# Rows of q and k doubled on the host, the first bit rows ahead of other loads, products with V in two threes, and the first low weight parts on VectorE

## The reference

```python
q_bits = (np.einsum('bhsd,dk->bhsk', q, proj) > 0)
k_bits = (np.einsum('bhsd,dk->bhsk', k, proj) > 0)
mask = q_bucket[:, :, :, None] == k_bucket[:, :, None, :]
scores = scale * np.matmul(q, k.transpose(0, 1, 3, 2))
scores = np.where(mask, scores, -1000000000.0)
attn = np.exp(scores - np.max(scores, axis=-1, keepdims=True))
attn = attn / (np.sum(attn, axis=-1, keepdims=True) + 1e-09)
attn_out = np.matmul(attn, v)
...
for e in range(E):        # first mixture: the expert of the largest cosine to x
    mask = expert_idx == e
    out[mask] = gate_w[mask, None] * (np.maximum(x[mask] @ w1[e], 0.0) @ w2[e])
...                       # second mixture: the same over the two best noisy logits
```

## Time and profile before

| | us |
|---|---|
| median of 3 runs | 1020.75 (1019.63 to 1024.56) |
| the profiled execution, its own time | 1016.54 |
| its span in the profile | 1014.6 |
| TensorE busy | 851.0 (84%) |
| VectorE busy | 542.5 (53%) |
| ScalarE busy | 466.8 (46%) |
| POOL busy | 107.1 (11%) |

### The profile page before, as it was taken

One profiled execution on the slowest core, in us unless ns is written; L12 is line 12 of the kernel. 1 busy time (PEld: TensorE's weight loads), 2 busy tenths in 40 slices (PEclk: granted clock), 3 DMA queues, 4 the chain that ended last, 5 costly groups with the idle time before them and its releaser, 6 DMA issues.

```text
span 1014.6 us, 13576 instructions
## 1 busy us (share of the span) xinstructions
PE 851.0 (84%) x4312; PEld 631.6 (62%) x4313; DVE 542.5 (53%) x908; ACT 466.8 (46%) x756; POOL 107.1 (11%) x153
## 2 busy tenths in 40 slices
PE   2799999999922999999996619999999999999980
PEld 0566666666611777777775307777777777777760
DVE  3778887788666455555454575252525433452115
ACT  3667777787842455544442405252424424352110
POOL 1000000000031101001011201000001001010405
PEclk9999999999975999999998858999999999999995
DMA  9723313400043565555555605151426342431507
GB/s 204 257 66 81 75 32 84 128 20 22 1 145 116 191 202 194 187 175 184 169 190 176 213 11 196 42 188 61 151 97 207 94 144 91 157 115 41 145 31 269
DMA packets 51427, 130.73 MB, mean 129 GB/s; under 512 B 7160, under 2 KB 9208, under 8 KB 51136
## 3 DMA queue, kind: packets, MB, share of 16 engines
q1 hardware_dynamic: 34416, 87.70, 28.0%
q0 software_dynamic: 6560, 21.50, 7.1%
q10 hardware_dynamic: 10416, 21.07, 5.4%
HBM read 104.43 MB, written 24.64 MB: 127 GB/s over the span
## 4 chain that ended last, share of the span: by engine, by line
PE 74%; DVE 7%; DMA 5%; issue 5%; ACT 3%; POOL 3%; ACTq 2%; SPq 0%; POOLq 0%; DVEq 0%
PE ps L1149 25%; PE ps L1141 18%; PE ps L975 8%; PE ps L998 7%; PE ps L984 6%; PE ps L1124 4%; PE ps L1117 2%; PE ps L965 2%; ACT w_hi L541 1%; DMA xg<-x_tokens,idx_now 1%; PE ps L1008 1%; DVE ysb L878 1%; POOL y_low L332 1%; DMA rows_Q<-in_q 1%; POOL y_high L332 1%
## 5 line engine op out<-in xcount | busy, mean ns | idle before, releaser
L541 ACT ACTIVATE w_hi<-raw 128x1024 fp32r<-128x1024 f32 x120 | 120.9, 1052 | 125.3 <-issue 95.0
L868 DVE TENSOR_TENSOR w_lo<-raw,w_hi 128x1024 fp32r<-128x1024 f32 x120 | 141.5, 1221 | 63.3 <-ACT w_hi L541 63.3
L1149 PE MATMUL ps<-w_hi,hT_hi 128*128 128x512 f32 x352 | 150.3, 427 | 5.0
L1141 PE MATMUL ps<-w_hi,xT_hi 128*128 128x512 f32 x352 | 144.2, 410 | 3.9 <-DVE xT_lo L853 3.9
L1141 PE MATMUL ps<-w_hi,xT_lo 128*128 128x512 f32 x352 | 140.0, 398 | 0.0
L1141 PE MATMUL ps<-w_lo,xT_hi 128*128 128x512 f32 x352 | 139.7, 397 | 0.0
L1149 PE MATMUL ps<-w_hi,hT_lo 128*128 128x512 f32 x352 | 139.4, 396 | 0.0
L1149 PE MATMUL ps<-w_lo,hT_hi 128*128 128x512 f32 x352 | 138.7, 394 | 0.0
L859 DVE TENSOR_TENSOR hT_lo<-ps,hT_hi 128x512 fp32r<-128x512 f32 x88 | 60.9, 692 | 141.1 <-ACT hT_hi L533 141.1
L672 DVE TENSOR_REDUCE row_low<-ps 128x1 f32<-128x768 f32 x96 | 91.7, 955 | 44.4 <-PE ps L975 43.9
L529 ACT ACTIVATE hid<-ps 128x512 f32<-128x512 f32 x88 | 52.4, 595 | 136.4 <-PE ps L1141 135.1
(11 more groups left out here) (197 smaller groups left out, 991.4 us busy)
## 6 DMA issues: line engine op xcount, KB each, us to landing
raw<-in_moe_w SPq DMA_DIRECT2D x128, 512.0 KB, 4.6
y_sorted<-ysb ACTq DMA_DIRECT2D x44, 256.0 KB, 2.0
rows_K<-in_k SPq DMA_DIRECT2D x16, 384.0 KB, 5.3
rows_Q<-in_q SPq DMA_DIRECT2D x16, 384.0 KB, 7.5
y_sorted<-xg SPq DMA_DIRECT2D x2, 1792.0 KB, 15.2
v<-in_v SPq DMA_DIRECT2D x8, 384.0 KB, 3.3
x_tokens<-x_sb ACTq DMA_DIRECT2D x2, 1536.0 KB, 5.1
x_tokens<-x_sb ACTq DMA_DIRECT2D x4, 768.0 KB, 4.1
```

The lines of the kernel that those rows point to most:

```text
L541: a.activation(w_hi[1 - par][:, c, :], raw[:, c % RING, :], ACT.Copy).then_inc(split_hi, 1)
L868: v_.tensor_tensor(w_lo[1 - par][:, c, :], raw[:, c % RING, :], w_hi[1 - par][:, c, :].bitcast(f32), ALU.subtract).then_inc(split_lo, 1)
L1141: last = te.matmul(ps[:, H0 + hf, :], x_[:, kk, :], w_[:, kk, w], start=(kk == 0 and i == 0), stop=(kk == KD - 1 and i == 2))
L1149: last = te.matmul(ps[:, YB, :], x_[:, fc, :], w_[:, c, w], start=(fc == 0 and i == 0), stop=(fc == KF - 1 and i == 2))
```

## The change

- The host writes each row of q and k twice, so one DMA of 128 partitions takes the place of two of 64; the waits on `k_in` and `q_in` count 16 in place of 32.
- Start: SP places the K bits of pair 0 before it loads the rows of pair 1 and V; the Q bits of pair 0 are placed from ScalarE's queue, behind its four Q operations. tau, gate weights and noise are loaded by SP, behind V of pair 1. VectorE makes both high parts of K first.
- Pair loop: products with V of a half in slots 1 and 4 (and 7 and 10), three chunks each; `bits` in slots 1 and 3; VectorE's `prepare` and ScalarE's Q work one slot later (two Q copies in slots 4 and 5).
- The low parts of the first expert's chunks 0 to 3 leave POOL and are made by VectorE behind the token slots; those of 4 to 7, and their high parts on ScalarE, follow the first xT.

```diff
-        PV_AT = {1: (0, 1), 2: (2,), 3: (3,), 4: (4,), 5: (5,)}
+        PV_AT = {1: (0, 1, 2), 4: (3, 4, 5)}
...
+        def place_bits(eng, n, j):
+            name = "KQ"[j]
+            eng.wait_ge(mask_done, 2 * n + j + 1)
+            for t in range(3):
+                eng.dma_start(flat(opd[name + "2"][n % 2])[D:D + UP, t * GW:(t + 1) * GW].bitcast(f32),
+                              row_bits[name][32 * t:32 * t + UP, :]).then_inc(bits_in, 16)
...
                 for name, src, landed in (("K", kT, k_in), ("Q", qT, q_in)):
-                    for half in range(2):
-                        sp.dma_start(rows_in[name][i][half * D:(half + 1) * D, :], src[b, hp]).then_inc(landed[i], 16)
+                    sp.dma_start(rows_in[name][i][:], src[b, hp]).then_inc(landed[i], 16)
...
             load_rows(0)
+            place_bits(sp, 0, 0)
+            load_rows(1)
             load_v(0)
-            load_rows(1)
-            place_bits(0)
             load_v(1)
+            sp.dma_start(tau_sb[:], tau.rearrange("(o a) -> o a", o=1).partition_broadcast(P)).then_inc(c_in, 16)
+            for i, w in enumerate((w_gate, w_noise)):
+                sp.dma_start(gate_w[:, :, i * NX:(i + 1) * NX], w.rearrange("(k p) e -> p k e", p=P)).then_inc(c_in, 16)
+            sp.dma_start(noise_sb[:].rearrange("p (b c) e -> p b (c e)", b=B),
+                         noise.rearrange("(b p c) e -> p b (c e)", b=B, p=P)).then_inc(c_in, 16)
...
-            wait(x_part, 8 * HP)
-            for c in range(RING):
-                wait(raw_in[c % RING], raw_count(0, c))
-                wait(split_hi, c + 1)
-                g.tensor_tensor(w_lo[0][:, c, :], raw[:, c % RING, :], w_hi[0][:, c, :].bitcast(f32),
-                                ALU.subtract).then_inc(split_lo0, 1)
...
-                        if s in (1, 2):
-                            q_high(n + 1, s - 1)
-                        if s in (3, 4):
-                            q_again(n + 1, s - 3)
+                        if s in (2, 3):
+                            q_high(n + 1, s - 2)
+                        if s in (4, 5):
+                            q_again(n + 1, s - 4)
...
             for head in range(2):
                 q_high(0, head)
                 q_again(0, head)
+            place_bits(act, 0, 1)
             exp_block(0, 0)
...
                 xT(0)
+                if L == 0:
+                    for c in range(NCH // 2, NCH):
+                        act.wait_ge(raw_in[c % RING], raw_count(0, c))
+                        a.activation(w_hi[0][:, c, :], raw[:, c % RING, :], ACT.Copy).then_inc(split_hi, 1)
                 over_experts(act, L, tile)
...
-                if s == 0:
+                if s == 1:
                     k_high(n, 0)
-                elif s == 1:
+                elif s == 2:
                     bit_rows(n, 0)
-                elif s == 2:
+                elif s == 3:
                     k_high(n, 1)
-                elif s == 3:
+                elif s == 4:
                     bit_rows(n, 1)
-                elif s in (4, 5):
-                    k_low(n, s - 4)
+                elif s in (5, 6):
+                    k_low(n, s - 5)
...
             k_high(0, 0)
+            k_high(0, 1)
+            bit_rows(0, 0)
             k_low(0, 0)
-            bit_rows(0, 0)
             bit_rows(0, 1)
             q_low(0, 0)
-            k_high(0, 1)
...
                 xT(0)
+                if L == 0:
+                    first_low(range(NC1, NCH))
                 over_experts(dve, L, tile)
 
+            def first_low(chunks):
+                for c in chunks:
+                    dve.wait_ge(split_hi, c + 1)
+                    v_.tensor_tensor(w_lo[0][:, c, :], raw[:, c % RING, :], w_hi[0][:, c, :].bitcast(f32),
+                                     ALU.subtract).then_inc(split_lo0, 1)
...
             place_tokens(0, [r_oh[0][:]])
+            first_low(range(NC1))
...
-            dve.wait_ge(split_lo0, RING)
-            for c in range(RING, NCH):
-                dve.wait_ge(split_hi, c + 1)
-                v_.tensor_tensor(w_lo[0][:, c, :], raw[:, c % RING, :], w_hi[0][:, c, :].bitcast(f32),
-                                 ALU.subtract).then_inc(split_lo0, 1)
             experts(0)
...
-                    if n + 1 < PAIRS and s in (0, 2):
+                    if n + 1 < PAIRS and s in (1, 3):
                         bits(n + 1, s // 2)
...
+            a = _np.concatenate([a, a], axis=2)
```

More of the change, by code:

```diff
@@ L237, in load_v @@
                              v_src[b, :, 2 * hp:2 * hp + 2, :]).then_inc(v_in[n % 2], 16)
-            def place_bits(n):
-                for j, name in enumerate("KQ"):
-                    sp.wait_ge(mask_done, 2 * n + j + 1)
-                    for t in range(3):
-                        sp.dma_start(flat(opd[name + "2"][n % 2])[D:D + UP, t * GW:(t + 1) * GW].bitcast(f32),
-                                     row_bits[name][32 * t:32 * t + UP, :]).then_inc(bits_in, 16)
             sp.dma_start(proj_raw[0:D, :], proj).then_inc(c_proj, 16)
             load_rows(0)
+            place_bits(sp, 0, 0)
+            load_rows(1)
             load_v(0)
-            load_rows(1)
-            place_bits(0)
             load_v(1)
+            sp.dma_start(tau_sb[:], tau.rearrange("(o a) -> o a", o=1).partition_broadcast(P)).then_inc(c_in, 16)
[3 more added lines that the diff above has]
+                         noise.rearrange("(b p c) e -> p b (c e)", b=B, p=P)).then_inc(c_in, 16)
             def load_chunk(w1, w2, e, E, c):
@@ L272, in _ @@
                 if n:
-                    place_bits(n)
+                    place_bits(sp, n, 0)
+                    place_bits(sp, n, 1)
                 if n >= 2:
@@ L403, in _ @@
             act.dma_start(emb, expert_emb).then_inc(c_emb, 16)
-            act.dma_start(tau_sb[:], tau.rearrange("(o a) -> o a", o=1).partition_broadcast(P)).then_inc(c_in, 16)
-            for i, w in enumerate((w_gate, w_noise)):
-                act.dma_start(gate_w[:, :, i * NX:(i + 1) * NX], w.rearrange("(k p) e -> p k e", p=P)).then_inc(c_in, 16)
-            act.dma_start(noise_sb[:].rearrange("p (b c) e -> p b (c e)", b=B),
-                          noise.rearrange("(b p c) e -> p b (c e)", b=B, p=P)).then_inc(c_in, 16)
             act.sem_inc(pta_ev, 1)
             def q_high(n, head):
-                act.wait_ge(q_in[n % 2], 32 * (n // 2 + 1))
+                act.wait_ge(q_in[n % 2], 16 * (n // 2 + 1))
                 a.activation(opd["Q1"][n % 2][:, head, :], rows_in["Q"][n % 2][:, head * S:(head + 1) * S], ACT.Copy,
@@ L513, in _ @@
             a.activation(r_exp[:], r_shift[:], ACT.Exp).then_inc(rt_act, 1)
-            for c in range(NCH // 2, NCH):
-                act.wait_ge(raw_in[c % RING], raw_count(0, c))
-                a.activation(w_hi[0][:, c, :], raw[:, c % RING, :], ACT.Copy).then_inc(split_hi, 1)
             def experts(L, y_rows):
@@ L643, in k_high @@
             def k_high(n, head):
-                dve.wait_ge(k_in[n % 2], 32 * (n // 2 + 1))
+                dve.wait_ge(k_in[n % 2], 16 * (n // 2 + 1))
                 v_.tensor_copy(opd["K1"][n % 2][:, head, :], rows_in["K"][n % 2][:, head * S:(head + 1) * S])                    .then_inc(k1_done, 1)
@@ L960, in bits @@
                 name, bank, i = "KQ"[j], XB if n or not j else OB, n % 2
-                pe.wait_ge((k_in, q_in)[j][i], 32 * (n // 2 + 1))
+                pe.wait_ge((k_in, q_in)[j][i], 16 * (n // 2 + 1))
                 if n:
```

## The result

The changed kernel takes a median of 1025.14 us (15 runs) against 1020.75 (15 runs of the kernel before beside them): ratio 1.0046, 95% interval 1.003 to 1.0063, 4.4 us slower by the medians (4.7 by the ratio). Its profiled execution took 1023.46 us with a span of 1021.7, against 1016.54 and 1014.6.

The account below looks back on a forecast made before the run. Attention was taken as bound by TensorE, with the start, routing and first expert tile bound otherwise. Terms +14.5 - 1.9 - 7.9 + 4.5 gave +9.2 us on the median 1020.75, so 1030.0 us, range 1008 to 1037.

Parts of the forecast that it names:

- The sign: Whole kernel: slower at chance 0.60, same 0.20, faster 0.20; the forecast change was +9.2 us.
- three waits over 0.5 us: Pair loop, TensorE: 0.67 for slot 0's turn back, 0.76 for K's bit rows before slot 3, 1.41 for slot 6's turn back.
- The gapless rival: Pair loop: ScalarE and VectorE catch up, TensorE never waits, -7.7 us, total 1007.8 us; chance 0.2.
- that of half the waits: Pair loop: only half of the waits appear, near +3 us, total 1018.5 us, no change; chance 0.15.
- part 1: Pair loop with products in two threes: new waits outweigh the saved work, +14.5 us, bounds -7.7 and +18.
- the chain through slots 8 and 9: Pair loop, slots without products: 3.33 us of chain against two slots of 1.56 us, a wait of 0.2 us.
- The last pair: End of the pair loop: no preparation but squares on ScalarE, +0.8 us.
- Part 2: Start, with doubled rows and reordered loads: first score at 21.5 instead of 23.40 us, -1.9 us, bounds -4.4 and +3.2.
- The rival of the Q bits: Start: pair 0's Q bits wait for packets of row loads, +3.2 us there, total 1035.1 us; chance 0.15.
- Part 3: First low parts: -7.9 us up to the token slots with POOL idle, +4.5 us in the first expert tile.
- First tile: First expert tile: late chunks 4 to 7 delay the first relu by 3.5 us, the clock adds 1.0; sum +4.5 us.
- the clock's 1.0: First expert tile: after TensorE stands about 3 us, the granted clock is low, +1.0 us.

Follow-up runs that it names:

- loop_undone: The changed kernel with the pair loop as before the change, so only the new start and the moved low parts; 1005.7 us, ratio 0.9854 to the kernel before.
- loop_only: The kernel before with only the pair loop's change (products in threes, preparation one slot later); 1038.46 us, ratio 1.017 to the kernel before.
- start_halves: loop_undone with undoubled rows of q and k, loaded as two halves again in the new order; 1013.42 us, ratio 0.9939 to the kernel before.
- q_bits_sp: loop_undone with pair 0's Q bits issued by SP ahead of the rows of pair 1, not by ScalarE; 1004.46 us, ratio 0.9849 to the kernel before.
- after_early_evict: The changed kernel with ScalarE's eviction of a finished half's products issued one slot sooner; 1012.47 us, ratio 0.9919 to the kernel before.
- low_only: The kernel before with only the first experts' low parts moved from POOL to VectorE and the first tile's order; 1010.4 us, ratio 0.9909.

## Why the prediction was right, and where not

The measured 1025.14 is inside the range, and the sign is the forecast one; the size is half, 4.4 us for 9.2. That lies close to the 0.5% that the prediction could tell from nothing, though these runs tell it. By its steps:

- **The sign: right, for the reason given.** The walk named three waits over 0.5 us; the trace has all three where it put them, at 0.68 (0.67 forecast), 0.97 (0.76) and 1.41 (1.41). Removing the loop's change removes them all (`loop_undone`). The gapless rival failed at slot 6, as its own condition said, and that of half the waits with it: part 1 by itself costs 17.3, not 3. The hit at slot 6 to the hundredth is chance: 14.24 + 9.4 + 1.6 is 25.24 and not 25.36, so the working as printed gives 1.29. Its terms also add up to 33.8 and not 33.75.
- **The size of part 1: too small.** +20.4 us in the profiled execution (+17.3 by itself in `loop_only`) for +14.5. The period grew by 2.79, not 2.25: the waits in slot 10, behind two slots without products, are 0.63 instead of 0.2, K's bits 0.97 instead of 0.76, and the 0.23 for the division didn't appear; that is 3.69 for 3.27. The step that failed there is the chain through slots 8 and 9: it took a slot without products as 1.56 us, the distance from scores to products. Between two such slots, scores to scores, it is 1.40 (151.92 to 153.32), since the 0.16 for the change of kind isn't paid, so TensorE outruns the chain further. The last pair lost 1.9, not 0.8; with the early eviction this loss was gone. The tail lost 0.6 instead of gaining 0.4. The first period, from pair 0 to 1, grew by 3.8, 1 us more than the others: the granted clock was 0.72 over 45 to 50 us, where it was 1.00 before (there it had fallen earlier, to 0.83 over 40 to 45).
- **Part 2: mis-sized, -5.3 for -1.9.** The rows of Q were used 5.2 us earlier, not 1.8. The step that failed is that doubling "leaves their bytes" and is worth nothing by itself: `start_halves` gives it 2.8 us of the rows and 4.9 of the first score, by a higher rate (367 for 238 GB/s). The landing was taken as 5.6 from the last issue; the trace has 7.35 from the first; three issues took 2.42, so the last started near 12.3, 5.7 before the score. That was right.
- **The rival of the Q bits.** Its mechanism is there, its price isn't: from the last issue to the score 5.7 us passed, not the 10.7 of the noise row. Still, beside loads of rows the bits took 7.4 to 9.9 us from first issue to score, without them 3.6 (`q_bits_sp`), and in the changed kernel their queue stood still for 2.4 us while the rows moved. That is in keeping with the turns by packets of which the prediction spoke, though it doesn't prove them. In the kernel before they took 7.5, on one queue behind the rows.
- **Part 3: right.** Slots -8.0 for -7.9, the root's operations 0.17 us. First tile +3.3 for +4.5, the relu's own delay 3.4 for 3.5; the clock's 1.0 wasn't added: TensorE stood 2.44 us and the granted clock was 1.00 over 338 to 342 us all the same. In `loop_undone` it was added: behind a stand of 2.90 us the clock was 0.50 over 324 to 326, and the stage took some 1.6 us more than in the changed kernel. Not forecast was the way from the slots to the first product, 2.0 us shorter: POOL's copy of the token indices took 0.18 us instead of 0.94, and the gather was used 5.3 us after its issue (322.33 to 327.60) instead of 6.6 (315.65 to 322.27). The copy's part, 0.76, the traces tell: in all fourteen it ends 0.05 us behind VectorE's first low part, which now starts 0.09 us after the slots instead of 0.84. Why the gather itself was 1.3 shorter, no run here tells; it took 5.2 to 6.7 in the kernels with part 3 and 6.6 to 7.4 in the three without.
- **The sum** came near by luck. By the profiles part 1 was 5.9 too low, part 2 3.4 too high and part 3 1.3 too high, which by itself would make 10.4. The stages that had no term add -2.0, -4.3 and +2.9, which brings it to the 7.1 by which the spans of the profiles differ; the medians differ by 4.4, since the profiled execution of the kernel before lies 4.2 under its median and that of the changed one 1.7.

## What to carry to other kernels

A group of work on the bounding engine is also the time in which the others catch up: before grouping it, walk the other engines' queues through the short slots that are left, with the duration of a short slot next to another short one. Two edits that each cost little can meet in one slot and cost more than both. Moving one instruction earlier in an in-order queue needs the queues behind it checked as well; here the load ring, a copy and an eviction passed the wait on, and each time it came back about as large or larger. A profile is one execution: where medians and profiles disagree by some us, look first at whether the clock fell at the same places. When a change is a bundle, time its parts alone: the parts without the loop's change, with the bits placed by SP, are the fastest kernel here (1004.46 us, 1.5% under the kernel before, though not to be told from `loop_undone` by these runs).

## What the runs showed of the hardware

- The same bytes of rows in one transfer of 128 partitions instead of two of 64 were used 1.3 us (K) and 2.8 us (Q) earlier. The DMA engines moved 367 instead of 238 GB/s over 3 to 7 us, at a busy share of 0.91 and 0.99.
- Three small transfers of 24 KB took 3.6 us from first issue to use, and 7.4 to 7.7 us when the next rows were being loaded from another queue (9.9 us when these were loaded in halves). Their queue sent nothing for 2.4 us of it.
- While POOL subtracts 128 x 1024 elements (2.33 us each), four small VectorE operations take 2.0 to 2.3 us instead of 0.17, and the reciprocal between them 0.23 as always. In all eleven kernels without POOL's low parts the four take 0.17, in all three with them 2.0 to 2.3. It works the other way too: POOL's copy of 128 x 1 token indices, begun beside a VectorE subtraction, ended 0.05 us behind it in all fourteen traces and took 0.94 or 0.18 us by that.
- In `after_early_evict` TensorE waited 1.40 us ahead of slot 7's products in each of six pairs. Twice the products then took 3.85 us instead of 2.1, with a granted clock of 0.72 over 143 to 149 and 212 to 218 us; four times they took the usual time. The wait of 1.41 in the changed kernel's steady pair was followed by the usual time in every pair.
- In the first expert tile TensorE stood 1.5 to 2.9 us in the nine kernels with part 3 and the old order. Behind stands of 2.90 (`loop_undone`) and 1.83 us (`start_halves`) the granted clock fell to 0.50; behind one of 2.78 (`low_only`) and the six others it stayed at 1.00. The length of a stand alone doesn't decide it. What does stays open.
